# Fused attention and two feed-forward blocks on one core: the sums of the prologue moved to VectorE, and a new order of the weight splitting

## The chip, the cores and the metric

The kernel runs on one core of one Trainium2 chip. The metric is the device time of one execution in microseconds. All data are 32-bit floats; TensorE gets each operand of the feed-forward blocks as a high and a low part (three matmuls for one), so most of the work of the other engines is splitting.

## The reference

```python
q_d, k_d, v_d = means of 4 neighbouring tokens of q, k, v        # 576 -> 144 tokens
out_up = repeat(softmax(q_d k_d^T / 8) v_d, 4)
out_local = softmax(where(|i - j| < 4, q k^T / 8, -1e9)) v
x = (out_up + out_local)              # (4, 8, 576, 64) -> 2304 tokens x 512
h = x @ w_in                          # 512 x 2048
y = where(h > 0, h, exp(min(h, 0)) - 1) @ w_out                  # 2048 x 512
g = y @ w_gate; out = (g * sigmoid(g) * (y @ w_val)) @ w_out2    # 512 x 1536, 1536 x 512
```

## The kernel before, in words

Attention is cut into 48 units: 12 groups of 192 tokens (three to a batch) times 4 pairs of heads. For a unit u the engines do, in this order: sums of 4 tokens of q and, once for each batch and pair, of k (dve_pool_q, dve_pool_k, L501 and L496; for units 1 to 3 of the prologue pool_pool_k on GpSimd, L817 and L819); scores on TensorE (pe_scores: local windows L334, pooled L343); mask and row maximum on VectorE (dve_masked_max, L507 to L513); exponentials on ScalarE (act_exps, L668 and L672); normalising on VectorE (dve_normalise, L518 to L525); transposes on TensorE (L352, L356) and their copies on ScalarE (act_copies, L680, L683); outputs on TensorE (pe_outputs: L368 with the windows of v, L375 with the pooled v_pool); their sum on VectorE (dve_output, L530, L534); and the split of the result in a high part (act_x_high, L689) and a low part (dve_x_low, L540).

v_pool holds the sums of 4 rows of v. They are formed by DMA: a plain load of the first row and three DMAs issued by GpSimd that add the next rows to it (pool_add_rows, L833 and L835), each waiting for the one before. The sums of the next batch follow, likewise on GpSimd's queue.

The first feed-forward block runs in 112 steps: 7 tiles of tokens (two of 192, five of 384) times 16 chunks of 128 hidden columns. Step s has a hidden part (pe_hidden: 12 matmuls, x times w1), elu (exp on ScalarE L705, dve_elu on VectorE L571 and L573), the split of g (act_g_high L709, dve_g_low L578) and an accumulation (pe_accumulate, 12 matmuls, g times w2). TensorE runs hidden s+2 ahead of accumulation s. Hidden s needs elu s-2 done (two banks).

In the first tile the 32 weight pieces (128 x 512) of w1 and w2 are split as they come: SP loads a piece into its landing place (L890; piece i waits until the low part of piece i-7 is formed), act_weight_a (L714) forms the high part, dve_weight_low (L546) the low part. In step s of the loop ScalarE and VectorE both do pieces 6+2s and 7+2s. Hidden s waits for the low part of piece 2s-2, accumulation s for that of piece 2s+3.

The attention of the units from 4 on is strewn into these steps by slots, two to a step: slot 2s in front of accumulation s, slot 2s+1 behind it. S_SLOT places the scores, NORM_SLOT, T_SLOT and O_SLOT normalising, transposes and outputs. For units 5 to 7 they lie 6 slots (3 steps) apart, then 4. All order is written out by hand; each engine takes its list in order and waits on counting semaphores. SP's list goes by the same slots: the load of q and k of unit u+2 stands behind the scores of unit u+1, and the pieces of a step behind it.

Of the kernel before, what the change touches and what calls it, by code (L numbers as in the profile page):

```python
# [5 lines left out]
F32 = mybir.dt.float32  # L6
# [72 lines left out]
ALIASED = 26  # L79
# [17 lines left out]
SUMS_AT = {S_SLOT[u - 1] + 2: u for u in range(PROLOGUE + 1, UNITS)}  # L97
# [25 lines left out]
def build(nc, qT, kT, v_rows, v_windows, w1, w2, wg, wv, w3, outT):  # L123
    ctx = ExitStack()
    with ctx:
# [34 lines left out]
        row_max = ra("row_max", [P, 2, TILES + 1], F32)  # L160
        neg_max = ra("neg_max", [P, 2, TILES + 1], F32)
        row_sum = ra("row_sum", [P, 2, TILES + 1], F32)
        row_inv = ra("row_inv", [P, 2, TILES + 1], F32)
# [16 lines left out]
        k_halved = first("k_halved", [P, PROLOGUE - 1, SP, POOL // 2], F32)  # L180
# [46 lines left out]
        v_row_loaded, v_rows_added = sem("v_row_loaded"), sem("v_rows_added")  # L227
# [7 lines left out]
        k_half_sums = sem("k_half_sums")  # L235
        k_first_pooled = [sem(f"k_first_pooled{p}") for p in range(PAIRS)]
# [87 lines left out]
        def pe_scores(pe, u):  # L324
# [11 lines left out]
            if u < PROLOGUE:  # L336
                pe.wait_ge(k_first_pooled[p], 1)
            elif j == 0:
                pe.wait_ge(k_pooled, (a - 1) * PAIRS + p + 1)
# [20 lines left out]
        def pe_outputs(pe, u):  # L360
# [9 lines left out]
            pe.wait_ge(v_rows_added, 32 * (POOL * (a + 1) - 1))  # L370
# [87 lines left out]
        def _(pe):  # L458
            for u in range(PROLOGUE):
                pe_scores(pe, u)  # L460
            for u in range(PROLOGUE - 1):
                pe_transposes(pe, u)
                pe_outputs(pe, u)
            pe_transposes(pe, PROLOGUE - 1)
            pe_scores(pe, PROLOGUE)
            pe_hidden(pe, 0, range(0, 2))
            pe_outputs(pe, PROLOGUE - 1)
            pe_hidden(pe, 0, range(2, KC))
            pe_hidden(pe, 1)
# [20 lines left out]
        def dve_pool_k(dve, u):  # L490
            a, p = batch_of(u), pair_of(u)
            wait_qk(dve, u)
            done = k_first_pooled[p] if a == 0 else k_pooled
            if a > 0:
                dve.wait_ge(scores_done, u - PAIRS + 1)
            nc.vector.tensor_reduce(k_pool[:, p, :], by_token(k_home(u)), AXX, ALU.add).then_inc(done, 1)  # L496
# [6 lines left out]
        def dve_masked_max(dve, u):  # L503
            x, r = bank_x(u), u % 2
# [10 lines left out]
        def dve_normalise(dve, u):  # L515
            r = u % 2
# [36 lines left out]

        def dve_behind_low(dve, at):
# [49 lines left out]
        def _(dve):  # L604
# [60 lines left out]
        def act_exps(act, u):  # L665
            x, r, p = bank_x(u), u % 2, prob(u)
# [86 lines left out]
        def _(act):  # L753
# [9 lines left out]
            act_exps(act, 1)  # L763
            act_copies(act, 0)
            act_exps(act, 2)
            act_copies(act, 1)
            act_exps(act, 3)
            act_x_high(act, 0)
            act_copies(act, 2)
            act_weight_a(act, 0)  # L770
            act_x_high(act, 1)
            act_weight_a(act, 1)
            act_copies(act, 3)
            act_x_high(act, 2)
            act_weight_a(act, 2)
            act_weight_a(act, 3)
            act_x_high(act, 3)
            for s in range(2):
                act_weight_a(act, EARLY_A + s)
                act_elu(act, s)  # L780
                act_g_high(act, s)
                if s == 0:
                    act_exps(act, PROLOGUE)
# [30 lines left out]
        def pool_pool_k(pool, u):  # L814
            wait_qk(pool, u)
            k, halved = by_token(k_home(u)), k_halved[:, u - 1, :, :]
            nc.gpsimd.tensor_tensor(halved, k[..., 0:2], k[..., 2:4], ALU.add).then_inc(k_half_sums, 1)  # L817
            pool.wait_ge(k_half_sums, u)
            nc.gpsimd.tensor_tensor(k_pool[:, pair_of(u), :], halved[..., 0], halved[..., 1],  # L819
# [181 lines left out]
```

## Time and profile before

| | |
|---|---|
| runs | 1035.34 us median of 3 (1034.89 to 1036.14) |
| profiled execution | 1034.78 us, span 1032.8 us |
| TensorE busy | 993.3 us, 96% |
| VectorE busy | 441.2 us, 43% |
| ScalarE busy | 355.9 us, 34% |
| GpSimd busy | 84.8 us, 8% |
| clock granted to TensorE, mean | 0.998 |

Busy shares are means over the span. The page's slices (40, of 25.8 us each) show TensorE at 2, 7, 9, 8 tenths in the first four or so and at 9 after that, so the reading goes by stretches of time. PE is TensorE, DVE VectorE, ACT ScalarE, POOL GpSimd, SP the engine that issues most loads; a small q behind a name is the engine's instruction queue. "Idle before" names what ended the engine's idle time.

### The profile page before, as it was taken

How to read it: one execution, taken by the hardware profiler on the slowest of the kernel's cores; microseconds unless marked ns; L12 is line 12 of the kernel's file. 1: busy time of each engine (PE TensorE's matmuls, PEld its weight loads, DVE VectorE, ACT ScalarE, POOL GpSimd, SP SyncE). 2: the span in 40 equal slices, each digit the busy share in tenths (PEclk: the TensorE clock that was granted, in tenths of full speed). 3: DMA queues.
4: the chain of work that ended last, by engine and by line, in shares of the span. 5: the costliest groups of instructions: out<-in, count | busy, mean ns of one | idle time of the engine just before them, and what ended most of it. 6: DMA issues, size and time to landing. Idle time of an engine off the chain costs nothing.

```text
span 1032.8 us, 17199 instructions
## 1 busy us (share of the span) xinstructions
PE 993.3 (96%) x6816; PEld 918.1 (89%) x6816; DVE 441.2 (43%) x1145; ACT 355.9 (34%) x1001; POOL 84.8 (8%) x81
## 2 busy tenths in 40 slices
PE   2798999999999999999999999999999999999998
PEld 1587899999999999999999988888888888889997
DVE  2467665555655556555435233223222322322222
ACT  2455544444544444444335612122121212112112
POOL 3300020001100000000016710000000000000000
PEclk9999999999999999999999999999999999999999
DMA  8544242112501211110054500020020002001000
GB/s 209 104 115 145 68 87 54 41 45 57 104 26 29 70 43 42 51 42 18 2 181 131 191 1 1 1 74 1 1 74 1 1 1 73 1 1 37 1 1 36
DMA packets 47863, 55.65 MB, mean 54 GB/s; under 512 B 7024, under 2 KB 36816, under 8 KB 47784
## 3 DMA queue, kind: packets, MB, share of 16 engines
q1 hardware_dynamic: 37800, 50.11, 15.7%
q0 software_dynamic: 9984, 4.45, 3.3%
q8 instruction: 54, 0.88, 0.4%
q14 instruction: 25, 0.20, 0.1%
HBM read 45.08 MB, written 9.44 MB: 53 GB/s over the span
## 4 chain that ended last, share of the span: by engine, by line
PE 90%; DVE 4%; ACT 2%; DMA 2%; issue 1%; POOL 1%; SPq 0%; DVEq 0%; ACTq 0%
PE bank L389 28%; PE bank L391 27%; PE bank L390 27%; PE bank L368 2%; DMA v_pool<-v_rows 2%; PE bank L334 2%; DVE weights L546 2%; PE bank L352 2%; PE bank L343 1%; PE bank L356 1%; PE bank L375 1%; ACT prob L672 1%; DVE g_sb L573 1%; ACT weights L714 0%; POOL v_pool L835 0%
## 5 line engine op out<-in xcount | busy, mean ns | idle before, releaser
L389 PE MATMUL bank<-x_hl,weights 128*128 128x464 f32 (+3 forms) x928 | 326.2, 351 | 5.6 <-DVE weights L546 4.3
L391 PE MATMUL bank<-x_hl,weights 128*128 128x464 f32 (+3 forms) x928 | 321.8, 347 | 0.0
L390 PE MATMUL bank<-x_hl,weights 128*128 128x464 f32 (+3 forms) x928 | 321.6, 347 | 0.0
L389 PEld LDWEIGHTS bank<-x_hl,weights 128*128 128x128 f32 x928 | 176.4, 190 | 17.2 <-DVE weights L546 5.0
L390 PEld LDWEIGHTS bank<-x_hl,weights 128*128 128x128 f32 x928 | 176.6, 190 | 10.2
L391 PEld LDWEIGHTS bank<-x_hl,weights 128*128 128x128 f32 x928 | 176.3, 190 | 10.3
L389 PE MATMUL bank<-g_hl,weights 128*128 128x384 f32 (+1 forms) x448 | 147.1, 328 | 0.0
L391 PE MATMUL bank<-g_hl,weights 128*128 128x384 f32 (+1 forms) x448 | 142.5, 318 | 0.0
L390 PE MATMUL bank<-g_hl,weights 128*128 128x384 f32 (+1 forms) x448 | 142.3, 318 | 0.0
L591 DVE TENSOR_TENSOR u_sb<-bank,u_sb 128x464 f32<-128x464 f32 (+1 forms) x60 | 38.3, 638 | 201.3 <-ACT u_sb L736 201.3
L736 ACT ACTIVATE u_sb<-bank 128x464 f32<-128x464 f32 (+1 forms) x60 | 33.4, 557 | 197.3 <-PE bank L391 197.3
L709 ACT ACTIVATE g_hl<-g_sb 128x384 fp32r<-128x384 f32 (+1 forms) x112 | 53.7, 479 | 129.2 <-DVE g_sb L573 129.2
L571 DVE TENSOR_SCALAR g_sb<-g_sb 128x384 f32<-128x384 f32 (+1 forms) x112 | 41.3, 369 | 129.8 <-ACT g_sb L705 129.8
L389 PEld LDWEIGHTS bank<-g_hl,weights 128*128 128x128 f32 x448 | 84.8, 189 | 8.8 <-issue 8.5
L738 ACT ACTIVATE u_hl<-u_sb 128x464 fp32r<-128x464 f32 (+1 forms) x60 | 35.3, 589 | 158.8 <-DVE u_sb L594 158.8
L389 PE MATMUL bank<-u_hl,weights 128*128 128x464 f32 (+1 forms) x240 | 89.1, 371 | 0.0
L391 PE MATMUL bank<-u_hl,weights 128*128 128x464 f32 (+1 forms) x240 | 89.0, 371 | 0.0
L390 PE MATMUL bank<-u_hl,weights 128*128 128x464 f32 (+1 forms) x240 | 88.9, 371 | 0.0
L705 ACT ACTIVATE g_sb<-bank 128x384 f32<-128x384 f32 (+1 forms) x112 | 49.6, 442 | 103.1 <-PE bank L391 103.0
L391 PEld LDWEIGHTS bank<-g_hl,weights 128*128 128x128 f32 x448 | 85.0, 190 | 0.0
L390 PEld LDWEIGHTS bank<-g_hl,weights 128*128 128x128 f32 x448 | 84.9, 190 | 0.0
L578 DVE TENSOR_TENSOR g_hl<-g_sb,g_hl 128x384 fp32r<-128x384 f32 (+1 forms) x112 | 56.1, 501 | 40.5 <-ACT g_hl L709 40.5
(91 smaller groups left out, 1038.6 us busy)
## 6 DMA issues: line engine op xcount, KB each, us to landing
landing<-w SPq DMA_DIRECT2D x44, 256.0 KB, 3.2
v_win<-v_windows SPq DMA_DIRECT2D x46, 105.0 KB
q_sb<-qT SPq DMA_DIRECT2D x46, 96.0 KB, 2.0
v_pool<-v_rows POOLq DMA_DIRECT2D x30, 144.0 KB, 4.7
k_sb<-kT SPq DMA_DIRECT2D x14, 288.0 KB, 3.4
yT_scratch<-y_sb SPq DMA_DIRECT2D x20, 192.0 KB, 2.1
y_raw<-yT_scratch SPq DMA_DIRECT2D x4, 928.0 KB, 5.2
outT<-out_sb SPq DMA_DIRECT2D x16, 232.0 KB, 2.2
```

What stands on the lines that cost most here:

```text
L334: nc.tensor.matmul(x[rows, t * WIN:(t + 1) * WIN], q[rows, t * QT:(t + 1) * QT], k[rows, k0:k0 + WIN], start=True, stop=True)
L352: nc.tensor.transpose(x[0:WIN, t * P:(t + 1) * P], prob(u)[:, t * WIN:(t + 1) * WIN], ident[:, :])
L389: nc.tensor.matmul(out, w_hi, x_hi, start=first, stop=False)
L390: nc.tensor.matmul(out, w_hi, x_lo, start=False, stop=False)
L391: return nc.tensor.matmul(out, w_lo, x_hi, start=False, stop=last)
L571: nc.vector.tensor_scalar(g, g, 1.0, -1.0, ALU.min, ALU.add).then_inc(t_done, 1)
L578: nc.vector.tensor_tensor(g_part(s, 1), g_sb[:, s % 2, 0:width1(s // NF1)], g_part(s, 0).bitcast(F32), ALU.subtract).then_inc(g_lo_done, 1)
L591: nc.vector.tensor_tensor(u, gate[f % 2][:, 0:w], u, ALU.mult).then_inc(gs_done, 1)
L705: nc.scalar.activation(g_sb[:, s % 2, 0:n], hid[s % 2][:, 0:n], ACT.Exp).then_inc(e_done, 1)
L709: nc.scalar.activation(g_part(s, 0), g_sb[:, s % 2, 0:width1(s // NF1)], ACT.Copy).then_inc(g_hi_done, 1)
L736: nc.scalar.activation(u_sb[:, f % 2, 0:w], gate[f % 2][:, 0:w], ACT.Sigmoid).then_inc(sg_done, 1)
L738: nc.scalar.activation(u_hl[:, f % 2, 0, 0:w], u_sb[:, f % 2, 0:w], ACT.Copy).then_inc(u_hi_done, 1)
```

## The change

It has these parts:

- Prologue, k: units 1 to 3 get their k sums from VectorE (dve_pool_k), as unit 0; pool_pool_k and its buffer go.
- Prologue, v: the four rows of v of batch 0 are loaded plainly, one load for each pair, into v_raw; VectorE adds them (dve_pool_v, two additions each). GpSimd adds rows by DMA for batches 1 to 3 alone, and for batch 1 this now waits for outputs_done of 8.
- SP's list starts with q and k of units 0 to 3, then v_raw, v windows and weight pieces mixed.
- VectorE does the four maxima of the prologue earlier in its list; the row statistics have 4 places and not 2. TensorE does the scores of unit 4 behind hidden 0 and 1, and the outputs of units 2 and 3 later.
- ScalarE's pieces are two ahead: in step s pieces 8+2s and 9+2s. VectorE's stay 6+2s and 7+2s.
- In step s VectorE forms the low part of g of step s+1 first, before elu of step s+2 (before: that of step s+2, after the masked maximum). ScalarE forms the high part of g of step s+2 after the exponentials of the slot (before: ahead of them).
- The sums of q and k of unit u are formed in the slot of the scores of unit u-1 (before: one step later).
- Pieces of column 22 and up (before: 26 and up) wait for the end of the prologue, whose buffers lie in their place.

```diff
-SUMS_AT = {S_SLOT[u - 1] + 2: u for u in range(PROLOGUE + 1, UNITS)}
+SUMS_AT = {S_SLOT[u - 1]: u for u in range(PROLOGUE + 2, UNITS)}
...
-            pe.wait_ge(v_rows_added, 32 * (POOL * (a + 1) - 1))
+            if a == 0:
+                pe.wait_ge(v_pooled, p + 1)
+            else:
+                pe.wait_ge(v_rows_added, 32 * POOL * a)
...
+            pe_transposes(pe, 0)
+            pe_outputs(pe, 0)
+            pe_transposes(pe, 1)
+            pe_outputs(pe, 1)
+            pe_transposes(pe, 2)
+            pe_transposes(pe, 3)
+            pe_outputs(pe, 2)
+            pe_hidden(pe, 0, range(0, 2))
+            pe_outputs(pe, 3)
+            pe_hidden(pe, 0, range(2, 3))
+            pe_hidden(pe, 1, range(0, 3))
+            pe_hidden(pe, 0, range(3, 4))
+            pe_hidden(pe, 1, range(3, 4))
             pe_scores(pe, PROLOGUE)
...
+        def dve_pool_v(dve, p):
+            dve.wait_ge(v_raw_loaded[p], 16)
+            x = v_raw[:, p, :, :, :]
+            nc.vector.tensor_tensor(x[:, :, 0:2, :], x[:, :, 0:2, :], x[:, :, 2:4, :], ALU.add).then_inc(v_half_sums, 1)
+            dve.wait_ge(v_half_sums, p + 1)
+            nc.vector.tensor_tensor(v_pool[:, 0, p, :, :], x[:, :, 0, :], x[:, :, 1, :], ALU.add).then_inc(v_pooled, 1)
...
+            dve_pool_q(dve, 0)
             dve_pool_k(dve, 0)
-            dve_pool_q(dve, 0)
             dve_pool_q(dve, 1)
+            dve_pool_k(dve, 1)
             dve.wait_ge(masks_set, 6)
             dve_masked_max(dve, 0)
             dve_pool_q(dve, 2)
+            dve_pool_k(dve, 2)
             dve_masked_max(dve, 1)
             dve_pool_q(dve, 3)
+            dve_pool_k(dve, 3)
+            dve_masked_max(dve, 2)
             dve_normalise(dve, 0)
-            dve_masked_max(dve, 2)
+            dve_masked_max(dve, 3)
+            dve_pool_v(dve, 0)
             dve_normalise(dve, 1)
-            dve_masked_max(dve, 3)
+            dve_pool_v(dve, 1)
             dve_output(dve, 0)
             dve_normalise(dve, 2)
-            dve_pool_q(dve, 4)
+            dve_pool_v(dve, 2)
+            dve_normalise(dve, 3)
             dve_output(dve, 1)
             dve_x_low(dve, 0)
-            dve_normalise(dve, 3)
+            dve_pool_v(dve, 3)
             dve_weight_low(dve, 0)
             dve_x_low(dve, 1)
             dve_output(dve, 2)
             dve_weight_low(dve, 1)
             dve_x_low(dve, 2)
+            dve_output(dve, 3)
+            dve_x_low(dve, 3)
+            dve_pool_q(dve, 4)
             dve_weight_low(dve, 2)
...
+            dve_elu(dve, 0)
+            dve_weight_low(dve, 4)
             dve_masked_max(dve, 4)
...
+            dve_elu(dve, 1)
+            dve_pool_q(dve, 5)
+            dve_weight_low(dve, 5)
+            dve_g_low(dve, 0)
             for s in range(STEPS):
+                if s + 1 < STEPS:
+                    dve_g_low(dve, s + 1)
                 if s + 2 < STEPS:
                     dve_elu(dve, s + 2)
                 dve_even_slot(dve, 2 * s)
-                if s + 2 < STEPS:
-                    dve_g_low(dve, s + 2)
-                dve_behind_low(dve, 2 * s)
                 dve_odd_slot(dve, 2 * s + 1)
...
             for s in range(STEPS):
                 if s + 2 < STEPS:
                     act_elu(act, s + 2)
+                act_even_slot(act, 2 * s)
+                if s + 2 < STEPS:
                     act_g_high(act, s + 2)
-                act_even_slot(act, 2 * s)
                 act_odd_slot(act, 2 * s + 1)
-                for i in range(EARLY_A + 2 + 2 * s, min(EARLY_A + 4 + 2 * s, N_PIECES_A)):
+                for i in range(EARLY_A + 4 + 2 * s, min(EARLY_A + 6 + 2 * s, N_PIECES_A)):
                     act_weight_a(act, i)
...
         def pool_add_rows(pool, a, r):
 
-            if r == 0 and a >= 2:
-                pool.wait_ge(outputs_done, (a - 1) * THIRDS * PAIRS)
...
+            if r == 0:
+                pool.wait_ge(outputs_done, max(2 * PAIRS, (a - 1) * THIRDS * PAIRS))
```

## Rows read from the trace of the kernel before

**Rows 1.** Busy time by windows: stretch, length, busy us (instructions) of each engine, clock, DMA share, GB/s.
```profile
0.00:42.90 42.90, 16.41 (x161) 12.09 (x161) 13.62 (x52) 13.27 (x53) 16.09 (x25) 1.00 0.68 152
...
48.00:52.00 4.00, 4.00 (x19) 4.00 (x20) 2.17 (x8) 2.42 (x11) 0.90 (x2) 1.00 0.73 177
...
53.30:118.50 65.20, 56.58 (x589) 52.71 (x587) 45.71 (x142) 36.80 (x122) 0.20 (x1) 0.97 0.40 116
118.50:1032.80 914.30, 911.15 (x6016) 844.65 (x6014) 376.22 (x936) 301.45 (x811) 63.88 (x52) 1.00 0.15 44
```

**Rows 2.** Chain of work that ended last, in order: start us, us, what.
```profile
3.08 4.76 DMA v_pool<-v_rows
...
9.03 10.42 DMA v_pool<-v_rows
...
33.55 0.79 PE bank L352 x3
...
36.96 0.79 PE bank L352 x3
```

**Rows 3.** Waits of the first 52 us: who for whom, us, times, longest.
```profile
PE bank L343 <- POOL k_pool L819: 19.1, 3, 10.0
```

**Rows 4.** VectorE in order of time: start us, us, line, operation, shapes, idle before.
```profile
4.29 0.75 DVE L496 TENSOR_REDUCE k_pool<-k_sb 128x144 f32<-128x576 f32 x1 [3.27 <-DMA k_sb<-kT]
...
8.85 0.35 DVE L501 TENSOR_REDUCE q_pool<-q_first 128x48 f32<-128x192 f32 x1 [1.08 <-DMA k_first<-kT]
...
62.08 0.37 DVE L507 TENSOR_TENSOR prob<-bank,mask 128x210 f32<-128x210 f32 x1
...
65.20 1.29 DVE L546 TENSOR_TENSOR weights<-landing,weights 128x512 fp32r<-128x512 f32 x2 [1.79 <-ACT weights L714]
66.41 0.25 DVE L571 TENSOR_SCALAR g_sb<-g_sb 128x192 f32<-128x192 f32 x1
...
66.97 0.20 DVE L530 COPY o_pool<-bank 128x48 f32<-128x48 f32 x1
...
67.58 0.35 DVE L578 TENSOR_TENSOR g_hl<-g_sb,g_hl 128x192 fp32r<-128x192 f32 x1
68.09 0.36 DVE L540 TENSOR_TENSOR x_hl<-x_raw,x_hl 128x192 fp32r<-128x192 f32 x1 [0.16 <-ACT x_hl L689]
...
68.63 0.16 DVE L518 TENSOR_SCALAR row_inv<-row_sum 128x4 f32<-128x4 f32 x1
...
69.53 1.29 DVE L546 TENSOR_TENSOR weights<-landing,weights 128x512 fp32r<-128x512 f32 x2
...
74.70 0.37 DVE L507 TENSOR_TENSOR prob<-bank,mask 128x210 f32<-128x210 f32 x1
```

**Rows 5.** ScalarE in order of time, same columns.
```profile
63.17 0.38 ACT L668 ACTIVATE prob<-bank,neg_max 128x144 f32<-128x144 f32 x1 [0.61 <-DVE neg_max L513]
...
64.55 1.14 ACT L714 ACTIVATE weights<-landing 128x512 fp32r<-128x512 f32 x2
...
71.69 0.47 ACT L680 ACTIVATE probT<-bank 70x384 f32<-70x384 f32 x1
...
72.27 1.14 ACT L714 ACTIVATE weights<-landing 128x512 fp32r<-128x512 f32 x2
```

**Rows 6.** TensorE in order of time, same columns.
```profile
113.18 0.46 PE L343 MATMUL bank<-k_pool,q_pool 64*64 64x144 f32 x4 [1.81 <-DVE q_pool L501]
...
121.27 0.57 PE L368 MATMUL bank<-probT,v_win 70*64 70x64 f32 x12
...
128.81 0.57 PE L368 MATMUL bank<-probT,v_win 70*64 70x64 f32 x12
```

**Rows 7.** Windows again, the one stretch with a lower clock (0.83).
```profile
110.00:120.00 10.00, 8.19 (x81) 7.61 (x80) 6.38 (x22) 4.81 (x19) 0.00 (x0) 0.83 0.18 51
```

**Rows 8.** Weight pieces' loads (L890) from 40 to 110 us: issue to landing.
```profile
DMA to landing us min/median/max: 2.7/3.2/5.3
```

**Rows 9.** GpSimd in order of time: the adding DMAs of batch 2.
```profile
137.45 1.47 POOL L833 DMA_DIRECT2D v_pool<-v_rows  x2 [83.95 <-PE bank L375]
...
156.71 2.45 POOL L835 DMA_DIRECT2D v_pool<-v_rows  x2 [4.01 <-DMA v_pool<-v_rows]
```

More of the change, by code:

```diff
@@ L78 @@
 EARLY_A = 4
-ALIASED = 26
+ALIASED = 22
 PROLOGUE = PAIRS
@@ L179, in build @@
         v_win_first = first("v_win_first", [WIN, 2, TILES, P], F32)
-        k_halved = first("k_halved", [P, PROLOGUE - 1, SP, POOL // 2], F32)
+        v_raw = first("v_raw", [SPH, PAIRS, 2, POOL, P], F32)
         prob_first = first("prob_first", [P, PROLOGUE, SCORES], F32)
@@ L226, in build @@
         vwin_first_loaded = [sem(f"vwin_first_loaded{j}") for j in range(2)]
-        v_row_loaded, v_rows_added = sem("v_row_loaded"), sem("v_rows_added")
+        v_raw_loaded = [sem(f"v_raw_loaded{p}") for p in range(PAIRS)]
+        v_half_sums, v_pooled, v_rows_added = sem("v_half_sums"), sem("v_pooled"), sem("v_rows_added")
         piece_loaded = [sem(f"piece_loaded{j}") for j in range(LOADS)]
@@ L335, in pe_scores @@
                                      k[rows, k0:k0 + WIN], start=True, stop=True)
[L336 to L339, printed above, removed]
+            if j == 0:
+                pe.wait_ge(k_pooled, a * PAIRS + p + 1)
             pe.wait_ge(q_pooled, u + 1)
@@ L490, in dve_pool_k @@
         def dve_pool_k(dve, u):
-            a, p = batch_of(u), pair_of(u)
             wait_qk(dve, u)
[L493 to L496, printed above, removed]
+            wait(dve, scores_done, u - PAIRS + 1)
+            nc.vector.tensor_reduce(k_pool[:, pair_of(u), :], by_token(k_home(u)), AXX, ALU.add).then_inc(k_pooled, 1)
+        def dve_pool_v(dve, p):
[4 more added lines that the diff above has]
+            nc.vector.tensor_tensor(v_pool[:, 0, p, :, :], x[:, :, 0, :], x[:, :, 1, :], ALU.add).then_inc(v_pooled, 1)
         def dve_pool_q(dve, u):
@@ L763, in _ @@
             act_exps(act, 1)
+            act_exps(act, 2)
             act_copies(act, 0)
-            act_exps(act, 2)
+            act_exps(act, 3)
             act_copies(act, 1)
-            act_exps(act, 3)
+            act_weight_a(act, 0)
             act_x_high(act, 0)
             act_copies(act, 2)
-            act_weight_a(act, 0)
-            act_x_high(act, 1)
             act_weight_a(act, 1)
             act_copies(act, 3)
+            act_x_high(act, 1)
             act_x_high(act, 2)
             act_weight_a(act, 2)
+            act_x_high(act, 3)
             act_weight_a(act, 3)
[L777 to L783, printed above, removed]
+            act_weight_a(act, 4)
+            act_elu(act, 0)
+            act_weight_a(act, 5)
+            act_elu(act, 1)
+            act_exps(act, PROLOGUE)
+            act_g_high(act, 0)
+            act_weight_a(act, 6)
+            act_weight_a(act, 7)
+            act_g_high(act, 1)
             for s in range(STEPS):
@@ L810, in _ @@
                 act_out(act, t)
[L814 to L819, printed above, removed]
-                                    ALU.add).then_inc(k_first_pooled[pair_of(u)], 1)
-        def pool_add_rows(pool, a, r):
-            if r == 0 and a >= 2:
-                pool.wait_ge(outputs_done, (a - 1) * THIRDS * PAIRS)
-            if a == 0 and r == 1:
-                pool.wait_ge(v_row_loaded, 32)
-            else:
-                pool.wait_ge(v_rows_added, 32 * (a * POOL + r - 1))
+        def pool_add_rows(pool, a, r):
+            if r == 0:
+                pool.wait_ge(outputs_done, max(2 * PAIRS, (a - 1) * THIRDS * PAIRS))
+            wait(pool, v_rows_added, 32 * ((a - 1) * POOL + r))
             for h in range(2):
@@ L852, in _ @@
                                     base=0, pattern=[[-1, P]], channel_multiplier=1).then_inc(ident_set, 1)
-            for u in range(1, PROLOGUE):
-                pool_add_rows(pool, 0, u)
-                pool_pool_k(pool, u)
             for a in range(1, BATCH):
@@ L879, in load_vwin, with load_vraw @@
             sp.dma_start(vwin_home(u), v_windows[a, row, p, :, at:at + TILES, :]).then_inc(done, 16)
-        def load_v_first_row(sp):
-            for h in range(2):
-                sp.dma_start(v_pool[:, 0, :, h, :], v_rows[0, :, :, h, 0, :].rearrange("p k d -> k p d")).then_inc(v_row_loaded, 16)
+        def load_vraw(sp, p):
+            sp.dma_start(v_raw[:, p, :, :, :], v_rows[0, p]).then_inc(v_raw_loaded[p], 16)
         def load_piece_a(sp, i):
@@ L931, in _ @@
         def _(sp):
-            load_qk(sp, 0)
-            load_qk(sp, 1)
-            load_v_first_row(sp)
-            load_qk(sp, 2)
-            load_qk(sp, 3)
-            for u in range(PROLOGUE):
-                load_vwin(sp, u)
-                load_piece_a(sp, u)
+            for u in range(PROLOGUE):
+                load_qk(sp, u)
+            load_vraw(sp, 0)
+            load_vwin(sp, 0)
+            load_vraw(sp, 1)
+            load_vwin(sp, 1)
+            load_piece_a(sp, 0)
+            load_vraw(sp, 2)
+            load_vwin(sp, 2)
+            load_piece_a(sp, 1)
+            load_vraw(sp, 3)
+            load_vwin(sp, 3)
+            load_piece_a(sp, 2)
+            load_piece_a(sp, 3)
             load_qk(sp, 4)
```

31 lines of the change are left out of this document (7 added, 24 removed).

## The prediction

> **What bounds the kernel now.** I read the busy time by windows first [rows 1]. From 118.5 us on TensorE is busy for 911.15 of 914.30 us; it is the bound there and the change leaves its instructions alone. So all that the change can give lies before 118.5 us: 42.9 us of prologue in which TensorE works 16.41 us, 10.4 us in which the first hidden steps start up, and 65.2 us (53.3 to 118.5) in which TensorE works 56.58, so has holes of 8.6 us. Then the chain that ended last [rows 2] and the table of waits [rows 3]: the prologue hangs on GpSimd. Its adding DMAs for v_pool stand in the chain one behind the other (4.76 us for the plain row, 10.42 for the first added one), each k sum of pairs 1 to 3 is queued behind one on GpSimd, and TensorE's pooled scores (L343) wait 19.1 us for those sums. In the third stretch I read VectorE and ScalarE in order of time over three steps (one attention unit) [rows 4, 5]: elu ends at 62.08 and, three steps later, at 74.70, so a round takes 12.62 us. TensorE needs less: where it never waits, two steps with one unit take 128.81 - 121.27 = 7.54 us [rows 6]; a further step without attention is 24 matmuls at about 0.11 us, 2.7 us (an estimate: the unit's own matmuls are about 2.1 of the 7.54), so 10.2 us a round. The round is a loop between VectorE and ScalarE: ScalarE splits a weight piece that VectorE wants at once (VectorE waits from 63.3 to 65.20), and VectorE waits for ScalarE's high part of g before it can form the low part.
>
> **The prologue, part by part.** GpSimd's adds and k sums of batch 0 go. VectorE gets three more k sums (L496 is 0.75 us long, the next instruction starts 0.08 before its end: 0.67 each, 2.0 in all [rows 4]) and four dve_pool_v. These no row shows. Their two adds have 512 and 256 elements in a row; the nearest rows are L546 (512 elements, two in 1.21 us, so 0.60) and L507 (210 elements, 0.29): 0.6 + 0.34 by straight line between these, and about 0.1 for the wait of the second for the first, 1.06 each, 4.2 in all. Bounds: 0.9 (no wait) and 2.0 (each part as slow as two L546) each; no gain below that, since nothing here hides behind another instruction of the same engine. I take 1.06, because the shapes are ordinary for the engine.
>
> With GpSimd gone the chain is VectorE's own list. I walk it: k and q of unit 0 are there at 4.29 [rows 4]. Unit 1 lands at 6.4 as now. Unit 2 landed at 8.85 with 1.44 MB ahead of it and with it; now the 288 KB of v are no longer ahead, so about 8, and unit 3 (1.54 MB in all) about 9.3. From 6.44, in the order of the new list: sums of unit 1 0.94, masked max 0 0.98, sums 2 0.94, max 1, sums 3, max 2, normalise 0 (0.90), max 3: 14.1 us. pool_v 0, normalise 1, pool_v 1: 17.1. Output 0, normalise 2, pool_v 2, normalise 3: 20.5. Output 1, low part of x 0, pool_v 3, first weight piece: 22.9. There the other side takes over: transposes, ScalarE's copies and outputs of one unit take 36.96 - 33.55 = 3.4 us in line [rows 2], which I split as 1.3, 0.8 and 1.3; with normalise 0 at 13.1 and normalise 1 at 16.1, units 0 and 1 keep TensorE to 20.1, transposes of 2 and 3 to 22.5, outputs 2 to 23.8. x low 1 comes at 24.0, output 2 at 24.6. TensorE does half of hidden step 0 (6 matmuls at 0.21, the rate at which 19 start in 4 us before 52 us; the clock column reads 1.00 there too, so it does not tell this rate [rows 1]) to 25.5, outputs 3 to 26.8, and VectorE output 3 and x low 3 to 28.2. The rest of hidden 0 and 1 is 18 matmuls, 3.9 us, of which 12 lie under that wait: hidden 0 is complete at 30.0, hidden 1 at 30.7, scores 4 at 32.0. Elu of step 0 starts at 30.6. VectorE goes on: elu 0 31.1, weight piece, masked max 4 33.1, elu 1 33.7, sums of unit 5, a piece, g low 0 (waits for the exponentials of unit 4 on ScalarE) 35.3, g low 1 36.6, elu 2 37.2, normalise 4 and two pieces 39.3, elu 3 40.1, two pieces 41.3, and elu 4, which waits for ScalarE's pieces 10 and 11, at 43.05. Before it was at 62.08 [rows 4]. Gain so far: 19.0 us.
>
> The loads are moved forward on SP (8 for q and k, then v and weights mixed); issuing costs about 0.45 us each, so the twenty are out by 10 us. By bytes, pieces 0 to 3 are complete after 4.2 MB. From 4.29 to 8.85 us 1.06 MB came in, 230 GB/s; at that rate 21 us, v of pair 3 about 18. The walk wants v of pair 0 at 14.1 (about 11), of pair 3 at 21.3, piece 0 at 18.7 (about 14). Covered by 3 us; were the cover gone, each late us costs one.
>
> **The loop of steps 2 to 11.** New order: VectorE g low of the next step first, elu, masked max, x low, sums, normalise, two pieces; ScalarE exp, x high and exponentials, g high, copies, two pieces. From end of elu to end of the next:
> - step with scores: masked max and gap 1.09 (62.08 to 63.17), exponentials 1.38 (63.17 to 64.55), g high 0.27 (an estimate from the like-sized x low, 68.09 to 68.63 with the q sum behind it), two pieces 1.04 (1.14 long, the next starts 0.1 earlier), exp 0.36 (an estimate from the same), elu 0.57 = 4.71 (now 4.89).
> - step with outputs: VectorE alone: output 0.61, wait for x high 0.51, x low 0.28, normalise 0.90, pieces 1.21, g low 0.28, elu 0.57 = 4.36 (now 4.34; the sum of the next q moves to the step before, where VectorE waits anyway).
> - step with transposes: g high with its gap 0.38, copies 0.58 (71.69 to 72.27), pieces 1.04, exp 0.36, elu 0.57 = 2.93 (now 3.39).
> Sum 12.00 against 12.62 [rows 4, 5]. So ScalarE two pieces ahead does not make the loop TensorE's: VectorE waits for the piece no longer, but ScalarE itself now stands in the loop, with g high behind the exponentials and the next exp behind two pieces. Steps 2 to 7: 24.0; 8 to 11, with units closer together: 4.71, 4.36, 5.29 (copies and exponentials in one step), 2.96 (VectorE: normalise, pieces, g low, elu): 17.3. From there ScalarE has no pieces left, the loop takes 6.6 us for two steps and TensorE needs 7.5: TensorE becomes the bound. It starts accumulation 15 some 8.0 us behind elu 14. The wait of 1.81 us of L343 for the q sum, at 113.18 [rows 6], goes, as the sum is done one step earlier, and the lower clock behind it (0.83 in that stretch [rows 7]) goes with it. 43.05 + 41.3 + 8.0 = 92.35, against 118.5 now. The gain is 26.1, of it 7.1 since elu 4.
>
> Weight pieces have one step less to land. SP issues a pair behind scores or outputs of the same step, and median landing takes 3.2 us, the longest 5.3 [rows 8]. In the walk ScalarE wants the pair 3.7 us after issue behind scores and 2.4 behind outputs (where the exp behind it has 0.6 us to spare). I put down 0.3 a round, 0.8 in all; if nearly all land at 4.1, it is 1 to 1.5 a round, 4 in all.
>
> Batch 1's four adding DMAs now wait for outputs 7 (near 81 us). For batch 2 the first is issued at 137.45 and the last at 156.71, landed some 4.5 later, 24 us in all [rows 9]; so done at 105, wanted by outputs 12 near 118. Hidden by 12 us.
>
> **Sum.** The profiled execution took 1034.8 (span 1032.8 and 2.0 around it); less 26.1, plus 0.8, 1009.5. The median is 0.56 above it: 1010.
>
> **Rivals.** (a) TensorE-bound loop: if ScalarE and VectorE overlap better than I laid them (shorter exponentials' wait), a round falls to 10.2; 1.8 a round more over 3.3 rounds, 6 us: 1004. For it, that each engine alone has under 9.5 us of work a round; against it, the chain above, whose form gives the present 12.62 exactly. (b) The loop gives nothing: pieces land late and ScalarE stands still before them; the prologue's 19 alone, 1016. For it, the tight 2.4 us. (c) The prologue is bound by its loads or by dve_pool_v at its upper bound (4 x 0.9 more and late pieces): 19 shrinks to 8 to 13, so 1016 to 1021. (d) It gives nothing measurable, because TensorE waits as long for something the walk misses: 1035. (e) Slower: TensorE at its lower clock. At half rate a round is 20.4 us instead of 12.0. The row with 0.83 [rows 7] shows that a hole of 1.8 us can bring the lower of the two levels (1.2 GHz against 2.4); the new start has such holes round 33 to 35 us. The cost is 8.4 a round, so it decides from about three rounds at half rate on; all of steps 0 to 11 so would give 33 more, 1043. Against it, the 10 us at 0.83 [rows 7] account for 1.7 of the 2.0 us that the mean of 0.97 over 65.2 us [rows 1] lacks, so the rest of that stretch, with most of its 8.6 us of holes, ran at the full clock, and a TensorE at half rate would have no holes left. The Trainium skill (TensorE: Matmul & The Clock Gate, "HAM oscillation") says that a kernel which waits between its groups of matmuls falls back to half rate and pays the rise anew each time; by that rule the time would be that of (e), and in the stretch from 53.3 to 110 us the trace does not agree with it: 0.97 over the whole [rows 1].
>
> **How the numbers follow.** Forecast 0.55 (own range 1006 to 1013), (a) 0.12, (b) 0.20, (c) 0.06, (d) 0.03, (e) 0.04. A run can tell about 0.2% from no change. Faster 0.93, same 0.03, slower 0.04. The range takes most of (a) and (b): 1003 to 1018.
>
> **What would show it.** First hidden matmul near 24 us, elu of step 0 near 30.6, elu 4 near 43; VectorE without long holes from 6 to 23 us, dve_pool_v pairs at 1.06; round of 12.0 in which ScalarE has hardly any wait but for VectorE's elu; TensorE without holes from about 86 us; v_pool of batch 1 landed 12 us before its use. The prediction is wrong if v_raw or pieces show as releasers in the prologue, if ScalarE's pieces wait for DMA in the loop, or if the clock column falls.

## The result, and the profile after

The changed kernel takes 1016.85 us (median of 4 runs, 1015.6 to 1018.62) against 1035.12 us: 0.9827 of the time, 95% interval 0.9806 to 0.9848, so 18.3 us faster. The profiled execution took 1015.6 us with a span of 1012.9. The forecast was 1010, with 1003 to 1018 as its range. One execution of e8 below took 1255.75 us at a mean granted clock of 0.73; neither its time nor its trace is used.

The same windows as in [rows 1], cut behind TensorE's last hole, which ends at 90.17 us (before: 113.18) (stretch, length, busy us and instructions of TensorE, its weight loads, VectorE, ScalarE, GpSimd, then clock, DMA share, GB/s):

```profile
0.00:42.90 42.90, 34.10 (x271) 28.69 (x271) 30.51 (x95) 22.61 (x81) 1.41 (x9) 1.00 0.62 168
42.90:97.70 54.80, 51.01 (x558) 47.73 (x557) 41.13 (x130) 32.15 (x112) 6.48 (x6) 1.00 0.53 147
97.70:1012.90 915.20, 912.16 (x5991) 845.96 (x5990) 376.10 (x932) 296.31 (x810) 66.32 (x54) 1.00 0.16 44
```

TensorE works 34.1 us in the first 42.9 where it worked 16.4, and its last hole ends 23.0 us earlier:

```profile
90.17 0.57 PE L365 MATMUL bank<-probT,v_win 70*64 70x64 f32 x12 [1.19 <-ACT probT L698]
```

But count the instructions of the last row. It holds 5991 of them in 915.20 us; the corresponding row of before holds 6016 in 914.30, because it begins 2.77 us ahead of the same place in TensorE's list (121.27 - 118.5). In this stretch TensorE's own list is the same and it waits for nobody, yet with 25 instructions less it is 0.9 us longer. That is the lead to the missing part of the gain.

VectorE in the prologue and at the two marks of the forecast (start us, us, line, operation, shapes, idle before):

```profile
4.17 0.35 DVE L510 TENSOR_REDUCE q_pool<-q_sb 128x48 f32<-128x192 f32 x1 [3.15 <-DMA k_sb<-kT]
...
13.69 0.68 DVE L503 TENSOR_TENSOR v_raw<-v_raw 72x512 f32<-72x512 f32 x1
14.40 0.42 DVE L505 TENSOR_TENSOR v_pool<-v_raw 72x256 f32<-72x256 f32 x1
14.74 0.16 DVE L527 TENSOR_SCALAR row_inv<-row_sum 128x4 f32<-128x4 f32 x1
...
29.93 0.26 DVE L578 TENSOR_SCALAR g_sb<-g_sb 128x192 f32<-128x192 f32 x1 [0.85 <-ACT g_sb L720]
...
44.23 0.37 DVE L516 TENSOR_TENSOR prob<-bank,mask 128x210 f32<-128x210 f32 x1
```

The additions of dve_pool_v take 14.74 - 13.69 = 1.05 us a pair. Elu of step 0 starts at 29.93, elu of step 4 ends at 44.23 where it ended at 62.08 [rows 4]: 17.85 us are gained there. The waits of [rows 3] read now:

```profile
PE bank L340 <- DVE k_pool L498: 0.6, 2, 0.4
```

0.6 us instead of 19.1. The outputs on TensorE (L365, L368 in the kernel before) show the rest, first in the tile with 192 columns, then in one with 384; two steps lie between two lines:

```profile
97.71 0.57 PE L365 MATMUL bank<-probT,v_win 70*64 70x64 f32 x12
105.25 0.57 PE L365 MATMUL bank<-probT,v_win 70*64 70x64 f32 x12
...
244.89 0.57 PE L365 MATMUL bank<-probT,v_win 70*64 70x64 f32 x12
255.56 0.57 PE L365 MATMUL bank<-probT,v_win 70*64 70x64 f32 x12
```

and of before, the same two steps of the tile with 384 columns:

```profile
268.12 0.57 PE L368 MATMUL bank<-probT,v_win 70*64 70x64 f32 x12
278.69 0.57 PE L368 MATMUL bank<-probT,v_win 70*64 70x64 f32 x12
```

At the first pair the changed kernel leads by 121.27 - 97.71 = 23.56 us [rows 6]; two steps take 7.54 us in both. The lead grows to 24.06 by 142 us of the changed kernel. In the wide tiles two steps take 10.67 us instead of 10.57, and the lead falls by 0.1 in each pair of steps, to 21.04 at the last outputs, and to 19.9 at the end (the spans). Some 4.1 us are given back, nearly all of it in the 80 steps with 384 columns, in which neither kernel has a hole. By form of instruction, the matmuls with 384 columns are longer, first before, then after (busy us, mean ns):

```profile
L390 PE MATMUL bank<-x_hl,weights 128*128 128x384 f32 x320 | 107.0, 334 | 0.0
L390 PE MATMUL bank<-g_hl,weights 128*128 128x384 f32 x320 | 107.0, 334 | 0.0
```

```profile
L390 PE MATMUL bank<-x_hl,weights 128*128 128x384 f32 x320 | 108.2, 338 | 0.0
L390 PE MATMUL bank<-g_hl,weights 128*128 128x384 f32 x320 | 108.1, 338 | 0.0
```

In steps where nothing else lies between them, twelve of them start 0.1736 us apart before and 0.1755 to 0.1764 after. Those with 192 and with 464 columns take what they took. 1920 matmuls of 384 columns times 2.3 ns are 4.4 us. The plainest measure, used again below, is the time from elu of step 31, the last of the narrow tiles (start of its second instruction on VectorE), to the end of the span: 1032.8 - 171.7 = 861.1 us before, 1012.9 - 147.9 = 865.0 after.

### The profile page after: what moved, and what is told of

It reads as the page before. It is cut to its first block, busy times and chain, and to the rows that moved or that the text cites. A ratio compares the mean times of both kernels' runs of the same rounds, so it can differ in the third digit from the quotient of the medians.

```text
span 1012.9 us, 17204 instructions
## 1 busy us (share of the span) xinstructions
PE 997.3 (98%) x6816; PEld 922.4 (91%) x6816; DVE 447.7 (44%) x1156; ACT 351.1 (35%) x1001; POOL 74.2 (7%) x69
## 4 chain that ended last, share of the span: by engine, by line
PE 93%; DVE 3%; ACT 2%; DMA 1%; issue 1%; SPq 0%; DVEq 0%; ACTq 0%
PE bank L389 29%; PE bank L390 28%; PE bank L391 28%; PE bank L365 2%; PE bank L333 2%; PE bank L349 2%; PE bank L353 1%; PE bank L375 1%; PE bank L340 1%; DMA k_first<-kT 1%; ACT weights L729 1%; ACT prob L687 0%; DVE weights L555 0%; DVE g_sb L580 0%; DMA landing<-w 0%
## 5 line engine op out<-in xcount | busy, mean ns | idle before, releaser
L390 PEld LDWEIGHTS bank<-x_hl,weights 128*128 128x128 f32 x928 | 176.8, 191 | 10.2
```

Of the source, the lines that this page charges most:

```text
L390: nc.tensor.matmul(out, w_hi, x_lo, start=False, stop=False)
```

## The experiments

Two theories for the loss in the wide tiles. **Placement**: the row statistics grew from 2 to 4 places, four tensors of 32 bytes more, and all that lies behind them, x_hl and g_hl too, moved by 128 bytes. **Order**: VectorE and ScalarE now do their work at other moments, and by that slow TensorE's matmuls. The first two kernels tell them apart; the other two take the change in its halves.

### e1_before_shifted

```diff
-        row_max = ra("row_max", [P, 2, TILES + 1], F32)
+        row_max = ra("row_max", [P, 4, TILES + 1], F32)
...
```

(the same for neg_max, row_sum and row_inv, in the kernel before)

> The kernel before with one change: the four small tensors of row statistics get 4 places and not 2, so that all tensors behind them (x_raw, x_hl, g_hl, g_sb, y_sb) lie 128 bytes further on, as in the changed kernel. Theory 'placement': the matmuls with 384 columns start 0.176 us apart and not 0.1736 (two steps with one unit 10.66 us and not 10.56), and the whole is 4 us slower, 1039. Rival 'order' (the new order of VectorE and ScalarE disturbs TensorE's reads): nothing changes, 1035 and 10.56.

Measured: 1037.82 us against 1034.68, ratio 1.0035 (1.0022 to 1.0047). The by-form rows are those of the changed kernel:

```profile
L390 PE MATMUL bank<-g_hl,weights 128*128 128x384 f32 x320 | 108.1, 338 | 0.0
```

128 bytes cost the kernel before 3.1 us, of 4 expected, with nothing else changed. From elu of step 31 to the end it takes 865.3 us, with VectorE and ScalarE in the old order. 'Order' falls as the cause of this loss.

### e2_after_old_places

```diff
-        row_max = ra("row_max", [P, PROLOGUE, TILES + 1], F32)
...
+        ra.at += 4 * 32
         neg_scale = ra("neg_scale", [P, TILES + 1], F32)
...
         y_sb = ra("y_sb", [P, KC, WIDE1], F32)
+        row_max = ra("row_max", [P, PROLOGUE, TILES + 1], F32)
...
```

> The changed kernel with the same row statistics, but laid behind y_sb, so that x_raw to y_sb lie where they lay in the kernel before. 'Placement': two steps of a 384-column tile with one unit take 10.56 us again, the whole 4 us less than the changed kernel, 1012.7. 'Order': 1016.9 and 10.66 as in the changed kernel.

Measured: 1009.7 us against 1034.68, ratio 0.9762 (0.9744 to 0.978); the changed kernel stood at 0.9827. Twelve matmuls of 384 columns start 0.173 us apart again:

```profile
L391 PE MATMUL bank<-g_hl,weights 128*128 128x384 f32 x320 | 107.0, 334 | 0.0
```

The edits that the change is about are worth 25.0 us; the changed kernel lost some 7 of them by the medians. The two traces stand 5.9 us apart: 1.9 already at elu of step 31 (the start, which differs from run to run, see e7 and e9) and 4.0 from there to the end (861.0 against 865.0); these 4.0 are placement. All kernels from here on have the old placement, unless said. From elu of step 31 to the end each of them but e5 and e8 takes 861.0 or 861.1 us, whatever its order of the parts of g.

### e3_prologue_alone and e4_loop_alone

```diff
...
-                if s + 1 < STEPS:
-                    dve_g_low(dve, s + 1)
                 if s + 2 < STEPS:
                     dve_elu(dve, s + 2)
                 dve_even_slot(dve, 2 * s)
+                if s + 2 < STEPS:
+                    dve_g_low(dve, s + 2)
+                dve_behind_low(dve, 2 * s)
...
-                for i in range(EARLY_A + 4 + 2 * s, min(EARLY_A + 6 + 2 * s, N_PIECES_A)):
+                for i in range(EARLY_A + 2 + 2 * s, min(EARLY_A + 4 + 2 * s, N_PIECES_A)):
                     act_weight_a(act, i)
```

(e3, from e2; e3 also has the old places of the q and k sums, of the low part of g of step 1 and of ScalarE's high part of g, and no two pieces ahead of the loop. e4 makes the reverse edits in the kernel before, and reorders VectorE's instructions just ahead of the loop to suit)

> The new prologue (sums on VectorE, plain loads) with the loop as before (pieces 6+2s on ScalarE, low part of g in the same step, sums one step later), old placement. Theory of the prediction: the prologue's gain alone, 18 us of it seen at elu of step 4, so about 1017.5; a round of three steps takes 12.6 us. Rival (the two parts need each other, since without the loop's slack the gain of the prologue is lost again at its first waits): 1020 or more.

> The old prologue (adding DMAs and k sums on GpSimd) with the new loop. Theory: a round takes 11.95 to 12.0 us and not 12.62, and the wait of 1.8 us with its lower clock near step 14 goes; 6 us less than before, 1029. Rival: the loop's gain is only that its start is in step with the new prologue; alone it gives under 2 us, 1033 or more.

Measured: e3 1017.09 us (ratio 0.9822, 0.98 to 0.9845), e4 1028.34 (0.9943, 0.9929 to 0.9956), both against 1034.68. So the prologue gives 17.6 us and the loop 6.3, together 23.9, and both at once (e2) 25.0. They add up within the intervals, which are some 2.3 us wide to each side for e3, so neither rival holds. The four runs of e3 fall in two pairs, near 1014.5 and near 1020; its trace is of the slowest, and in it TensorE has a hole of 1.80 us up to 84.94 and then a granted clock of 0.50 from 85.9 to 96.0. Elu's second instruction on VectorE (0.28 us after its start elu ends) over one round, of e3 and of e4:

```profile
45.73 0.36 DVE L583 SCALAR_TENSOR_TENSOR g_sb<-bank,g_sb 128x192 f32<-128x192 f32 x1
...
58.36 0.36 DVE L583 SCALAR_TENSOR_TENSOR g_sb<-bank,g_sb 128x192 f32<-128x192 f32 x1
```

```profile
61.16 0.36 DVE L573 SCALAR_TENSOR_TENSOR g_sb<-bank,g_sb 128x192 f32<-128x192 f32 x1
...
73.65 0.36 DVE L573 SCALAR_TENSOR_TENSOR g_sb<-bank,g_sb 128x192 f32<-128x192 f32 x1
```

12.63 us in e3, as before. In e4 the first round takes 12.49 and the next ones 11.95, the value of the changed kernel.

### e5_g_shifted and e6_x256_g512

```diff
+        ra.at += 128
         g_hl = ra("g_hl", [P, G_RING, 2, WIDE1], F32R)
```

(e5; in e6 x_hl moves by 256 bytes and g_hl by 512)

> The changed kernel with the old placement of x_raw and x_hl, but g_hl, g_sb and y_sb 128 bytes further on. Theory 'the moving operand's own address': only the matmuls that read g_hl slow down (12 of 384 columns in 2.11 us instead of 2.08), those on x_hl stay at 2.08; the whole about 2 us above the 1009.7 of the old placement. Rival 'any tensor that the others write or the lay-out as a whole': both kinds slow down, or neither.

> As the changed kernel with the old placement, but x_hl 256 bytes further on and g_hl 512. If what counts is a multiple of 512 bytes (each row of 384 floats is 3 x 512 bytes, and both tensors began at the same place modulo 512 in the old placement), the matmuls on x_hl take 2.11 us for 12 and those on g_hl 2.08. If a multiple of 256 is enough, both 2.08; if the place modulo 1024 counts, g_hl slows too.

One execution each: 1012.92 and 1009.04 us. In e5 twelve matmuls on g_hl start 0.1764 us apart and twelve on x_hl 0.1727 to 0.1745. By form:

```profile
L392 PE MATMUL bank<-g_hl,weights 128*128 128x384 f32 x320 | 108.1, 338 | 0.0
...
L392 PE MATMUL bank<-x_hl,weights 128*128 128x384 f32 x320 | 107.4, 335 | 0.0
```

and in e6 both are fast:

```profile
L394 PE MATMUL bank<-x_hl,weights 128*128 128x384 f32 x320 | 107.1, 335 | 0.0
L394 PE MATMUL bank<-g_hl,weights 128*128 128x384 f32 x320 | 107.0, 334 | 0.0
```

So it is mainly the place of the moving operand's own tensor that counts: over all groups of twelve, disturbed ones included, the mean distance rises by 2.3 ns for g_hl in e5 (to 180.0) and by 0.7 for x_hl (to 177.4), where the changed kernel has 2.1 and 2.3 more. The 0.7 on the tensor that did not move is not explained. From elu of step 31 to the end e5 takes 863.7 us and e6 861.0. From the old place, 128 bytes on slow it, 256 and 512 do not. Of the cases put down for e6, the one in which 256 is enough came true; a step of 256 fits all four kernels. Why 128 bytes matter, and why nothing of it shows at 192 columns, stays open.

### e7_not_ahead

```diff
-            act_weight_a(act, 6)
-            act_weight_a(act, 7)
             act_g_high(act, 1)
...
-                for i in range(EARLY_A + 4 + 2 * s, min(EARLY_A + 6 + 2 * s, N_PIECES_A)):
+                for i in range(EARLY_A + 2 + 2 * s, min(EARLY_A + 4 + 2 * s, N_PIECES_A)):
                     act_weight_a(act, i)
```

> The changed kernel with old placement, but ScalarE's weight pieces in step with VectorE's (6+2s in step s), the low part of g still one step later. By the walk of the loop: step with scores 1.09 + 1.38 + 0.27 (g high) + 0.62 (one piece) + 1.21 + 0.28 + 0.57 = 5.4 us, with outputs 4.36, with transposes 3.6, a round 13.4 instead of 11.95; so 4 to 5 us slower than with pieces ahead, 1014.5. Rival (being ahead is worth nothing, since ScalarE has slack): 1009.7 and 11.95.

Measured: 1019.58 us against 1034.61, ratio 0.9852 (0.9825 to 0.9879), 9.9 us above e2. VectorE over one round:

```profile
46.09 0.36 DVE L581 SCALAR_TENSOR_TENSOR g_sb<-bank,g_sb 128x192 f32<-128x192 f32 x1
...
49.74 1.29 DVE L556 TENSOR_TENSOR weights<-landing,weights 128x512 fp32r<-128x512 f32 x2 [2.05 <-ACT weights L730]
...
57.73 1.29 DVE L556 TENSOR_TENSOR weights<-landing,weights 128x512 fp32r<-128x512 f32 x2 [1.54 <-ACT weights L730]
...
59.50 0.36 DVE L581 SCALAR_TENSOR_TENSOR g_sb<-bank,g_sb 128x192 f32<-128x192 f32 x1
```

The round is 13.41 us, the 13.4 of the walk. VectorE waits 2.05 and 1.54 us for ScalarE's piece: the high part of g behind the exponentials pushes the pieces back. The whole costs twice the expected 4 to 5 us. The traces of e7 and e2 stand 11.6 us apart. Elu 4 ends 4.2 us later (46.4 against 42.2), and 1.8 of that is there already at elu 0 (30.61 against 28.85), ahead of anything the edit moves: TensorE is at half rate there in e7 and at full rate in e2. Elu 0 of e7, then of e2:

```profile
30.61 0.36 DVE L581 SCALAR_TENSOR_TENSOR g_sb<-bank,g_sb 128x192 f32<-128x192 f32 x1
```

```profile
28.85 0.36 DVE L581 SCALAR_TENSOR_TENSOR g_sb<-bank,g_sb 128x192 f32<-128x192 f32 x1
```

From elu 4 to elu 14 e7 loses 3.8 us to e2; this is the part that the walk had priced, at 4 to 5. Another 3.6 come behind that, where TensorE has a hole of 3.07 us up to 87.65 and is at half rate from 92 to 96. So being ahead pays 3.8 us in the loop; how much of the rest is the edit's and how much the clock's was not separated.

### e8_g_order_old and e9_g_order_old_again

```diff
...
-                if s + 1 < STEPS:
-                    dve_g_low(dve, s + 1)
                 if s + 2 < STEPS:
                     dve_elu(dve, s + 2)
                 dve_even_slot(dve, 2 * s)
+                if s + 2 < STEPS:
+                    dve_g_low(dve, s + 2)
...
                     act_elu(act, s + 2)
-                act_even_slot(act, 2 * s)
-                if s + 2 < STEPS:
                     act_g_high(act, s + 2)
+                act_even_slot(act, 2 * s)
```

(pieces stay two ahead; the low part of g of step 1 moves ahead of the loop)

> The changed kernel with old placement and pieces two ahead, but the parts of g in the old order: high part before the exponentials of the slot, low part in the same step behind the masked maximum. By the walk: with scores 1.09 + 1.38 + 1.04 + 0.36 + 0.57 = 4.44 us (g high now lies in the gap ahead of the exponentials), with outputs 4.1 to 4.3, with transposes 2.93, a round 11.5 to 11.7; so 1 to 2 us faster, 1008.3. Rival (VectorE's stall of 0.5 us a step for the high part, which the move was to take away, comes back): a round of 12.6 or more, 1012 or more.

> The same kernel as e8_g_order_old, whose trace was disturbed, for an undisturbed trace. Theory (the walk of the loop): with scores 4.44 us from elu to elu, with outputs 4.1 to 4.3, with transposes 2.93; a round of 11.5 to 11.7 against 11.95, and the whole 1 to 2 us below the 1009.7 of the changed kernel at the old placement. Rival: a round of 12 or more, no difference in the whole.

Measured: e8 at a ratio of 0.975 (0.9727 to 0.9774), e9 1011.01 us, 0.9773 (0.9758 to 0.9789). e9, one round:

```profile
57.93 0.36 DVE L583 SCALAR_TENSOR_TENSOR g_sb<-bank,g_sb 128x192 f32<-128x192 f32 x1
62.36 0.36 DVE L583 SCALAR_TENSOR_TENSOR g_sb<-bank,g_sb 128x192 f32<-128x192 f32 x1
66.43 0.36 DVE L583 SCALAR_TENSOR_TENSOR g_sb<-bank,g_sb 128x192 f32<-128x192 f32 x1
69.36 0.36 DVE L583 SCALAR_TENSOR_TENSOR g_sb<-bank,g_sb 128x192 f32<-128x192 f32 x1
```

4.43, 4.07 and 2.93, together 11.43 us against 11.95: the new order of the parts of g is no gain but costs 0.5 us a round, once ScalarE is ahead. As to the whole, the theory is not borne out by these two: e8 is 0.1% below e2 and e9 0.1% above, both within the intervals. In e9 elu 4 ended at 45.9 and not at 42.2. TensorE was at half rate from 24 to 32 us and again from 36 to 42 (clock 0.51), in e2 from 34 to 37 only:

```profile
36.00:42.00 6.00, 6.00 (x31) 6.00 (x30) 3.90 (x12) 2.15 (x7) 0.00 (x0) 0.51 0.24 83
```

### e10_fillers

```diff
+            pe.wait_ge(ident_set, 1)
+            fill(5)
             for u in range(PROLOGUE):
                 pe_scores(pe, u)
+            fill(3)
             pe_transposes(pe, 0)
+            fill(2)
             pe_outputs(pe, 0)
             pe_transposes(pe, 1)
+            fill(2)
             pe_outputs(pe, 1)
```

(fill(n) are n matmuls of the identity with itself into a bank that is free then)

> The changed kernel at the old placement with 12 additional matmuls of 128 x 128 on the identity (results unused) in TensorE's list of the prologue: 5 ahead of the first scores, 3 ahead of the transposes of unit 0, 2 behind the transposes of unit 0 and of unit 1. Theory (the late start of elu 4, 1.2 us behind the forecast, comes from TensorE still at its lower rate until 35 to 39 us, because it works with holes before): the matmuls of hidden 0 and 1 start 0.11 us apart and not 0.21, elu 4 ends 2 to 3 us earlier, the whole about 1007, with less spread. Rival (the fillers come too early to matter, or only delay the scores and transposes): elu 4 where it was or up to 1 us later, 1010.

Measured: 1011.14 us against 1035.02, ratio 0.9777 (0.9761 to 0.9792): no gain. TensorE does leave the half rate early: its transposes take 0.49 us from 13.15 us on, as at full rate, and 0.85 in e2. But the pace of that stretch is VectorE's list, TensorE gets a hole of 1.25 us at 19.3, and from 22.85 to 29.1 it is at half rate again: the matmuls of hidden 0 and 1 start 0.21 us apart, while in e2, without fillers, they start 0.11 apart. So what the theory asks for in hidden 0 and 1 did not come about, and the run does not decide what a full rate there is worth. Elu 4 ends at 41.6, 0.5 us earlier, not 2 to 3. And then ScalarE waits for a weight piece:

```profile
44.10 0.35 ACT L734 ACTIVATE g_hl<-g_sb 128x192 fp32r<-128x192 f32 x1
46.46 1.29 ACT L739 ACTIVATE weights<-landing 128x512 fp32r<-128x512 f32 x2 [2.02 <-DMA landing<-w]
```

The pieces were issued at 41.88, behind the scores of unit 5, and landed 4.6 us later. Three more such waits of 0.50 to 0.57 us follow; the first round from elu 4 on takes 14.22 us and the next 12.55, where e2 has 12.64 and 11.95. This is the mechanism of rival (b): pieces that land late.

### e11_k_on_gpsimd

```diff
             dve_pool_q(dve, 1)
-            dve_pool_k(dve, 1)
...
+            for u in range(1, PROLOGUE):
+                pool_pool_k(pool, u)
             for a in range(1, BATCH):
                 for r in range(POOL):
                     pool_add_rows(pool, a, r)
```

> The changed kernel at the old placement, but the k sums of units 1 to 3 on GpSimd as before (2.05 us each), with the v rows still by plain loads and VectorE's additions. Theory (what cost the old prologue its time is the adding DMAs in GpSimd's queue, not where the k sums are formed): scores of unit 3 complete 1.5 to 2 us later than with the sums on VectorE (13 instead of 11.1), VectorE's list 2 us shorter; the whole within 1 us of 1009.7, at most 1.5 slower. Rival (the sums on VectorE are a main part of the gain): 5 us or more slower, 1015.

Measured: 1009.59 us against 1035.02, ratio 0.9767 (0.9745 to 0.9789), the same as e2. The k sums on VectorE are not what gives the gain; what cost was their place behind the adding DMAs on GpSimd. And GpSimd was quicker than I had put down:

```profile
6.39 0.67 POOL L840 TENSOR_TENSOR k_halved<-k_sb 128x288 f32<-128x288 f32 x1 [4.07 <-DMA k_sb<-kT]
7.14 0.42 POOL L842 TENSOR_TENSOR k_pool<-k_halved 128x144 f32<-128x144 f32 x1
```

In the kernel before the same instruction took 1.63 us, right behind the issue of two adding DMAs:

```profile
8.15 2.56 POOL L835 DMA_DIRECT2D v_pool<-v_rows  x2 [5.83 <-DMA v_pool<-v_rows]
9.77 1.63 POOL L817 TENSOR_TENSOR k_halved<-k_sb 128x288 f32<-128x288 f32 x1
```

### e12_all_together

```diff
+            for i in range(LOADS, LOADS + 2):
+                load_piece_a(sp, i)
             load_qk(sp, 6)
...
+                for i in range(LOADS + 2 + 2 * s, min(LOADS + 4 + 2 * s, N_PIECES_A)):
+                    load_piece_a(sp, i)
                 sp_slot(sp, 2 * s)
                 sp_slot(sp, 2 * s + 1)
-                for i in range(LOADS + 2 * s, min(LOADS + 2 + 2 * s, N_PIECES_A)):
-                    load_piece_a(sp, i)
```

(on top of the edits of e8 and e11)

> The changed kernel at the old placement with three edits: the parts of g in the old order (as in e8 and e9), the k sums of units 1 to 3 on GpSimd (as in e11), and the loads of a step's weight pieces issued one step earlier, ahead of the slot's waits in SP's list. Theory: ScalarE no longer waits for landing pieces in the loop (2.6 us in 5 waits in e2 between 20 and 90 us, 2.9 in e9), a round takes 11.4 us, elu 4 ends near 41 to 42 where the low clock does not last, and the whole is 2 to 3 us below the 1009.7 of e2: 1007. Rival (the start is set by TensorE's low clock, whose end varies from run to run, and eats what the loop gives): 1009 to 1011 as e2, e9 and e11.

Measured: 1006.91 us (5 runs, 1005.21 to 1007.27) against 1034.01, ratio 0.9727 (0.9711 to 0.9742). It is the fastest of all, 2.8 us below e2 and some 10 below the changed kernel. ScalarE's waits from 20 to 90 us have no line for landing pieces any more; e2's have:

```profile
ACT weights L730 <- DMA landing<-w: 2.6, 5, 0.7
```

The round is 11.42 us and elu 4 ends at 41.97. Which of its three edits gives how much of the 2.8 us was not taken apart in the time; by the rounds (0.52 us each over some 3.4 rounds, an estimate) 1.8 of it is the order of g.

## Why the prediction was right where it was, and what it missed

The measured 1016.85 lies in the range, 6.9 above the 1010 of the forecast, outside its own narrower range of 1006 to 1013. The mechanism held, but that the number lies in the range is in part luck: the upper end of 1018 was taken for rival (b), and what filled it was a cost that no rival named. By its time alone the result would have passed for (b), 1016. Point by point:

- **What bounds, and what the prologue gains.** Right. Elu 0 was forecast at 30.6 and starts at 29.93. The walk put VectorE's list up to the maximum of unit 3 at 14.1, it is done at 13.7; dve_pool_v at 1.06, it is 1.05; unit 3 landed at 9.9 and not 9.3, and cost 0.1 us. But for that the loads were not the bound here (in e2 TensorE waits 0.66 us for the same load). e3 gives the prologue 17.6 us.
- **Elu 4 at 43.05.** It ended at 44.23, 1.18 us late. I let TensorE go at half rate in hidden 0 and 1 only. It stayed there until 38.9 us, though it worked 18.2 of the 18.9 us from 20 on, and hidden 3, then the transposes of unit 4, and by them ScalarE's pieces, came late. In the other kernels the end of this stretch lies elsewhere (see below), so the term has a spread of 3 to 5 us that the forecast did not have.
- **The loop.** Right to a few hundredths: a round of 11.95 against 12.00, and 41.8 us for steps 4 to 14 against 41.3. The first round took 12.51, 0.3 of it for a piece that landed late. e7 (13.4 forecast, 13.41 measured) and e9 (11.5 to 11.7 forecast, 11.43 measured) bear the same arithmetic out at two other orders, e9 to 0.1 us.
- **TensorE as bound from step 12 on, the wait of L343 and the low clock gone.** Right: the changed kernel leads by 23.56 us at the first common pair, by 24.06 soon after. With the 0.8 for landing the forecast said 25.3. TensorE's last hole, forecast to end about 86, ended at 90.17; it is one of 1.19 us, for ScalarE's copies of the transposes (L698), which the walk did not have.
- **Batch 1's adding DMAs behind outputs 7.** Right: issued from 82.37 to 100.81 us, landed near 108, outputs 12 at 120.33.
- **What was missed.** The step that failed is a sentence at its start: "the change leaves its instructions alone". It does, but not their operands' places. The diff shows four tensors that grow and a list in which each tensor begins where the last one ends. I priced the edit at nothing without naming it. It costs 4.1 us in the trace (24.06 to 19.9), 3.1 in e1.

The sum: 1010, plus 1.18 (elu 4), plus 0.1 (loop and landing), plus 4.1 (placement), plus 0.7 (2.7 us around the span and not 2.0), plus 0.7 (the median lies 1.25 above the profiled execution and not 0.56) gives 1016.8.

Of the rivals, (a) is out: no order tried comes to 10.2 a round. (b) was wrong as put, since the loop gave 6.3 us alone, but its mechanism is there, 1.0 us of waits in the changed kernel, 2.6 in e2, 2.0 in one piece in e10. (c) and (d) are out by e3. (e) did not come: there is some low clock in each start, the longest later stretches last some 10 us (e3 from 86 to 96, e1 from 101 to 111), and it costs a few us, not 33.

## What to carry to other kernels

When a buffer is resized in a list of tensors laid one behind the other, say what moves, and compare the duration of an unchanged instruction in a stretch where nothing waits; here it found 4 us beside a gain of 18. In a loop of two engines, write the chain from one fixed event to the next for each kind of step: it told the round of three orders to 0.1 us, where the engines' busy shares (each under 9.5 us a round) would have told of a bound that is never reached. And loads that stand in the issuing queue behind a wait for the bound engine lose their lead as soon as that engine is no longer late.

## What the runs showed of the hardware that was not expected

- A matmul of 128 x 128 on 384 moving columns starts 0.1736 us behind the last one or 0.1755 to 0.1764, by where its moving operand begins: 128 bytes beyond the old place is slow, 0, 256 and 512 are fast (e1, e2, e5, e6). It goes mainly by the tensor's own place; e5 has a small rise, 0.7 ns, on the tensor that did not move. With 192 and 464 columns no difference was seen; the tensors of the 464-column phase did not move. The Trainium skill (SBUF — State Buffer, "Operand start alignment") has a rule on which starts are legal, multiples of the element size, and says of its measurements that they timed nothing; 128 bytes keep that rule and still cost 1.3% of the matmul's pace here.
- Kernels with the same lists for TensorE stand at different rates in the first 45 us. In the changed kernel TensorE is at half rate (0.213 us between matmuls of 192 columns, 0.111 at full rate) up to 38.9 us, though it worked 18.2 of the 18.9 us before that:

```profile
38.53 0.41 PE L390 MATMUL bank<-x_hl,weights 128*128 128x192 f32 x1
38.74 0.33 PE L391 MATMUL bank<-x_hl,weights 128*128 128x192 f32 x1
38.91 0.27 PE L389 MATMUL bank<-x_hl,weights 128*128 128x192 f32 x1
```

  In e2 it is at full rate from 23.9, then waits 2.25 us (up to 33.15) for the low part of g of step 0 and is at half rate from 34 to 37; in e9 it is low from 24 to 32 and from 36 to 42; in e10 it stays at full rate behind a hole of 2.24 us that ends at 34.12. Elu 4 ends at 41 to 46 us in the kernels with the new prologue, latest in e3, e7 and e9, where TensorE is at half rate for 14 to 17 us between 23 us and there, and at 41.1 in e11, with 3 us of it. The clock column shows the later drops (0.83 and 0.88 in e2) but reads 1.00 in the first stretch at half rate.

```profile
30.00:36.00 6.00, 3.75 (x26) 3.61 (x25) 4.45 (x17) 4.34 (x16) 0.00 (x0) 0.83 0.68 210
36.00:42.00 6.00, 6.00 (x58) 5.70 (x57) 3.70 (x10) 2.95 (x8) 0.00 (x0) 0.88 0.00 0
```

- GpSimd's addition of 128 x 288 took 1.61 to 1.63 us right behind the issue of its own adding DMAs (before) and 0.66 to 0.68 without them (e11). Why is not shown; the profile's spans on GpSimd are rough.
